# Splitting the next expert's weights in two steps in a routed mixture-of-experts stage

## The chip, the cores and the metric

The kernel runs on one core of a Trainium2 chip. The metric is the device time of one execution in microseconds (us); lower is better. The engines are PE (matrix products), DVE (vector), ACT (scalar), POOL (GpSimd) and SP, which here only issues DMAs.

## What is computed

Three parts follow one another: an mLSTM-like attention over 2 x 768 tokens, a dense mixture of four experts, and a routed mixture of eight experts. The change lies in the last one:

```python
def _moe2_ref(x, w_gate, w1, w2, capacity):
    N, D = x.shape                      # 1536, 320
    E = w_gate.shape[1]                 # 8
    logits = x @ w_gate
    expert_idx = np.argmax(logits, axis=1)
    ...                                 # gate_w: softmax probability of the chosen expert
    disp = np.zeros((E, capacity, D))   # capacity 384
    ...                                 # each token is copied to the next free row of its expert
    h = np.maximum(np.einsum('ecd,edf->ecf', disp, w1), 0.0)   # F = 1024
    y = np.einsum('ecf,efd->ecd', h, w2)
    ...                                 # out[i] = gate_w[i] * y[expert, row]
```

## The kernel before

**Precision by splitting.** Products run in a reduced format. Each operand is therefore held as a high part and a low part (value less high part), and three products are summed: high x high, low x high, high x low. The weights are split on the chip, each expert's while the expert before it is computed.

**Staging.** SP loads the weights of an expert in four pieces into `stage` (704 KB each, one buffer per piece), and a piece is loaded again as soon as POOL has counted it done on `w_ready`. Per piece p the split has these steps, in order of dependence:

- ACT, `w_to_hi`, two parts: the high part of w1 (L762, 128x768) and of w2 (L765, 128x640). Part number 2p is w1, 2p + 1 is w2.
- DVE, `w_tail`: the low part of a corner of w1, in place (L1151, 64x256), and with `w2_share` the low part of the first of the piece's two w2 tiles (L1155, 128x320). Both read `stage` and a high part, both in SBUF. It counts on `w_tail_done`.
- POOL, `w_to_lo`: waits for `w_tail_done`, then subtracts the rest of w1 (L897, 128x512) and, with `skip=1`, the other w2 tile (L905, 128x320), and counts on `w_ready`. PE waits for `w_ready` of piece p ahead of up tile 2p of the next expert.

**One routed expert.** Buffers alternate by parity (even, odd). PE makes 8 up tiles (f = 0 to 7, eight products each, L509 to L512), into three PSUM banks by turns: from f = 3 it waits until DVE has made h_lo of tile f - 3. ACT takes each tile as h_hi (L770), DVE as h_lo (L1186). At f = 3, 5 and 7 (`SLOT_STEPS`) PE also transposes a tile of the next expert's token rows (L638), which ACT (L833) and DVE (L1310) take over; after the last of them DVE waits for `out_sent` of the expert before and copies gates and token numbers (L1317, L1318). Then come the down products, 24 for each tile of 128 tokens, in the order of `TILE_ORDER` (2, 1, 0). DVE evicts each tile (L1332), POOL sends it with an indirect DMA (L1022). The three sends stand on POOL behind the four pieces of the next expert's weights. Tiles with no tokens are left out on PE, by a count in a register; DVE and POOL go through all three in every case, and PE signals the missing ones at once (a transpose, L678, stands in for one). With at most two tiles of tokens the up products are 256 columns wide, else 384.

In this run the experts, numbered here from 0, have 3, 1, 1, 1, 3, 3, 2 and 2 tiles. The routed stage's first up product starts at 468.66 us.

**The order of the work around the change** is written out by hand: each engine runs its own list, and a step stands where the code puts it. On DVE the steps of the weights stand after f = 1, 3, 5 and 7 (`W_STEPS`), on ACT one part after each f.

Of the kernel before, what the change touches and what calls it, by code (L numbers as in the profile page):

```python
# [41 lines left out]
def build_kernel(nc, gates, o_tok, q_t, qk_t, kv_tok, probs, w_moe1, w_moe2, w_gate, out, capacity):  # L42
# [8 lines left out]
    E1 = w_moe1.shape[0]  # L51
    E2 = w_moe2.shape[0]
    PIECES, STAGE = w_moe1.shape[1], w_moe1.shape[3]
# [5 lines left out]
    PF = F // PIECES  # L59
# [21 lines left out]

    SLOT_STEPS = (3, 5, 7)

    W_STEPS = (1, 3, 5, 7)

    SHIFTED, CHOSEN, SLOTS = 2, 5, 14
    LAST1 = BLOCKS1 - 1
# [14 lines left out]
    with ExitStack() as ctx:  # L102
# [126 lines left out]
        def xs_bank(e, par, n):  # L229


            if isinstance(e, int) and e == 0:
                return bank[7 - n]
            return bank[7 - (par + n) % 2]
# [473 lines left out]
        def _(act):  # L708
# [48 lines left out]
            def w_to_hi(x, w, p, part):  # L757


                if part == 0:  # L760
                    act.wait_ge(stage_in[p], 16 * x + 16)
                    act.activation(w1_hi[w][:, :, p * PF:(p + 1) * PF],  # L762
                                   stage[:, p, 0:KT * PF].rearrange("p (k f) -> p k f", k=KT), ACT.Copy).then_inc(w_hi_done, 1)
                else:
                    act.activation(w2_hi[w][:, p * PK:(p + 1) * PK, :],  # L765
                                   stage[:, p, KT * PF:STAGE].rearrange("p (k d) -> p k d", k=PK), ACT.Copy).then_inc(w_hi_done, 1)

            def hidden_hi(g, f):
                act.wait_ge(h_psum, 8 * g + (f + 1))
                act.activation(h_hi[:, f, :], ps_h[f % 3][:, 0:BLOCK], ACT.Relu).then_inc(h_hi_done, 1)  # L770
# [44 lines left out]
            e = E1 - 1  # L815
# [15 lines left out]
            def slots_to_hi(e, par, n):  # L831
                act.wait_ge(xs_psum, 3 * e + (n + 1))
                act.activation(xs_hi[par][:, :, n * P:(n + 1) * P], xs_bank(e, par, n)[:, 0:XD].rearrange("p (k t) -> p k t", k=KT),  # L833
                               ACT.Copy).then_inc(xs_hi_done, 1)

            def routed(e, par, last):
                for f in range(FT):
                    hidden_hi(e + G1, f)
                    if not last:
                        if f in SLOT_STEPS:  # L840
                            slots_to_hi(e + 1, 1 - par, SLOT_STEPS.index(f))
                        w_to_hi(e + (E1 + 1), 1 - par, f // 2, f % 2)

            for n in range(NT):
                slots_to_hi(0, 0, n)
            with act.Fori(0, E2 // 2 - 1) as i:
                routed(2 * i, 0, False)
                routed(2 * i + 1, 1, False)
            routed(E2 - 2, 0, False)
            routed(E2 - 1, 1, True)  # L850

# [185 lines left out]
        def _(dve):  # L1037
# [108 lines left out]
            def w_tail(x, w, p, cols, w2_share=False):  # L1146


                dve.wait_ge(w_hi_done, 8 * x + (2 * p + 1))
                hi = w1_hi[w][TAIL:P, 2, cols]  # L1150
                op = dve.tensor_tensor(hi, stage[TAIL:P, p, 2 * PF:3 * PF], hi.bitcast(F32), ALU.subtract)  # L1151
                if w2_share:
                    dve.wait_ge(w_hi_done, 8 * x + (2 * p + 2))
                    raw = stage[:, p, KT * PF:KT * PF + X]
                    op = dve.tensor_tensor(w2_lo[w][:, p * PK, :], raw, w2_hi[w][:, p * PK, :].bitcast(F32), ALU.subtract)  # L1155
                op.then_inc(w_tail_done, 1)
# [27 lines left out]
            def hidden_lo(g, f):  # L1184
                dve.wait_ge(h_hi_done, 8 * g + (f + 1))
                dve.scalar_tensor_tensor(h_lo[:, f, :], ps_h[f % 3][:, 0:BLOCK], 0.0, h_hi[:, f, :].bitcast(F32),  # L1186
                                         ALU.max, ALU.subtract).then_inc(h_done, 1)
# [86 lines left out]
            e = E1 - 1  # L1274
# [32 lines left out]
            def slots_to_lo(e, par, n):  # L1307
                cols = slice(n * P, (n + 1) * P)
                dve.wait_ge(xs_hi_done, 3 * e + (n + 1))
                dve.tensor_tensor(xs_lo[par][:, :, cols], xs_bank(e, par, n)[:, 0:XD].rearrange("p (k t) -> p k t", k=KT),  # L1310
                                  xs_hi[par][:, :, cols].bitcast(F32), ALU.subtract).then_inc(xs_done, 1)
                if n == NT - 1:
                    for k in range(NT):
                        dve.wait_ge(x_slot_in[par][k], 8 * e + (16 - 8 * par))

                    dve.wait_ge(out_sent[par], 24 * e - 24 * par)
                    dve.tensor_copy(gate_s[par][:], x_slot[par][:, :, GATE]).then_inc(meta_done, 1)  # L1317
                    dve.tensor_copy(token_s[par][:], x_slot[par][:, :, TOKEN]).then_inc(meta_done, 1)  # L1318

            def routed(e, par, last):  # L1320
                for f in range(FT):
                    hidden_lo(e + G1, f)
                    if not last:
                        if f in SLOT_STEPS:
                            slots_to_lo(e + 1, 1 - par, SLOT_STEPS.index(f))
                        if f in W_STEPS:
                            p = W_STEPS.index(f)
                            w_tail(e + (E1 + 1), 1 - par, p, slice(p * PF, (p + 1) * PF), w2_share=True)
                dve.wait_ge(meta_done, 2 * e + 2)
                for k, n in enumerate(TILE_ORDER):  # L1330
                    dve.wait_ge(y_psum, 3 * e + (3 * G1 + k + 1))
                    dve.tensor_scalar(y_out[par][:, n, :], ps_y[n][:, 0:X], gate_s[par][:, n:n + 1], None,  # L1332
                                      ALU.mult).then_inc(y_free, 1)

            for n in range(NT):
                slots_to_lo(0, 0, n)
            routed(0, 0, False)
            routed(1, 1, False)
            with dve.Fori(1, E2 // 2 - 1) as i:
                routed(2 * i, 0, False)  # L1340
                routed(2 * i + 1, 1, False)
# [59 lines left out]
```

## Time and profile before

| | us |
|---|---|
| median of 3 runs | 618.19 |
| the runs | 614.89, 619.23, 618.19 |
| the profiled execution, its own time | 620.88 |
| its span, first to last instruction | 619.1 |
| mean granted clock of PE over the span | 0.988 |

All rows below are from the profiled execution. The granted clock is 1.00 at 2.4 GHz and 0.50 at 1.2 GHz. A timeline row gives start, duration, engine, line of the code, operation, tile written <- tiles read, shapes, and in brackets the idle time before it and what ended it. PE rows overlap, since matrix products are pipelined; the distance between starts is what one costs.

### The profile page before, as it was taken

To read this page: it belongs to the slowest core of one execution; us is meant where nothing else is said; L and a number is where in the kernel's file an instruction comes from. 1 tells how busy PE (TensorE), PEld (TensorE's weight loads), DVE (VectorE), ACT (ScalarE), POOL (GpSimd) and SP (SyncE) were. 2 spreads that over 40 slices of the span, in tenths; PEclk is the share of its full clock that TensorE was granted. 3 is DMA by queue.
4 is the path that set the end of the run, shared out by engine and by line. 5 is a ranking of instruction groups with operands and counts; after the bars stand their busy time and mean duration, and the time that the engine had idled before them with its cause. 6 is when DMAs were issued, how large, how long until landed. Compare 5 with 4: busy or idle time off the path is not lost.

```text
span 619.1 us, 10721 instructions
## 1 busy us (share of the span) xinstructions
PE 585.3 (95%) x3847; PEld 571.0 (92%) x3847; DVE 284.9 (46%) x607; ACT 215.3 (35%) x468; POOL 212.6 (34%) x238
## 2 busy tenths in 40 slices
PE   0999999999999999999999999999988998899996
PEld 0877889999999999999999999999977998899996
DVE  7378876223322332332233232443434499855472
ACT  5344564213311321331132133131204286555341
POOL 9656539111101101110110121312331567764461
PEclk9999999999999999999999999999987999899999
DMA  6497634951011101101110110211123747764400
GB/s 193 112 231 180 164 146 138 365 213 47 0 47 48 47 0 47 47 1 47 47 47 0 48 47 1 86 42 45 60 70 107 237 156 238 246 220 143 158 16 18
DMA packets 25910, 63.50 MB, mean 103 GB/s; under 512 B 3310, under 2 KB 15543, under 8 KB 25876
## 3 DMA queue, kind: packets, MB, share of 16 engines
q1 hardware_dynamic: 23956, 58.98, 29.8%
q0 software_dynamic: 1920, 4.07, 1.8%
q8 instruction: 21, 0.34, 0.2%
q14 instruction: 13, 0.11, 0.1%
HBM read 52.16 MB, written 13.11 MB: 105 GB/s over the span
## 4 chain that ended last, share of the span: by engine, by line
PE 83%; POOL 4%; issue 3%; DVE 3%; ACT 3%; DMA 2%; SPq 1%; POOLq 0%; DVEq 0%; ACTq 0%
PE bank L509 27%; PE bank L524 9%; PE bank L525 9%; PE bank L526 9%; PE bank L512 5%; PE bank L511 4%; PE bank L667 3%; PE bank L666 3%; PE bank L665 3%; PE bank L447 2%; PE bank L475 2%; PE bank L579 1%; PE bank L568 1%; ACT h_hi L770 1%; POOL c_select L867 1%
## 5 line engine op out<-in xcount | busy, mean ns | idle before, releaser
L770 ACT ACTIVATE h_hi<-bank 128x384 fp32r<-128x384 f32 x192 | 94.7, 493 | 312.6 <-PE bank L512 311.9
L1186 DVE SCALAR_TENSOR_TENSOR h_lo<-bank,h_hi 128x384 fp32r<-128x384 f32 x192 | 105.7, 556 | 131.9 <-ACT h_hi L770 130.9
L897 POOL TENSOR_TENSOR w_lo_odd<-stage,w_hi_odd 128x512 fp32r<-128x512 f32 x24 | 31.4, 1307 | 149.0 <-DVE w_hi_odd L1151 119.6
L897 POOL TENSOR_TENSOR w_lo_even<-stage,w_hi_even 128x512 fp32r<-128x512 f32 x24 | 31.4, 1309 | 132.7 <-DVE w_hi_even L1151 119.6
L509 PE MATMUL bank<-xt_hi,w_hi_even 128*128 (+2 forms) x192 | 65.2, 340 | 3.4 <-DVE h_lo L1186 2.1
L509 PE MATMUL bank<-xt_hi,w_hi_odd 128*128 128x384 f32 (+2 forms) x192 | 63.6, 331 | 2.3 <-DVE h_lo L1186 2.3
L1195 DVE SCALAR_TENSOR_TENSOR acc<-bank,prob,acc 128x320 f32 (+1 forms) x36 | 19.8, 551 | 95.8 <-PE bank L526 92.9
L509 PE MATMUL bank<-xt_lo,w_hi_even 128*128 (+2 forms) x192 | 63.5, 331 | 0.0
L509 PE MATMUL bank<-xt_hi,w_lo_even 128*128 (+2 forms) x192 | 63.5, 331 | 0.0
L509 PE MATMUL bank<-xt_lo,w_hi_odd 128*128 128x384 f32 (+2 forms) x192 | 61.8, 322 | 0.0
L509 PE MATMUL bank<-xt_hi,w_lo_odd 128*128 128x384 f32 (+2 forms) x192 | 61.7, 322 | 0.0
L524 PE MATMUL bank<-w_hi_odd,h_hi 128*128 128x320 f32 x192 | 59.9, 312 | 0.0
L524 PE MATMUL bank<-w_hi_even,h_hi 128*128 128x320 f32 x192 | 59.4, 309 | 0.1
L525 PE MATMUL bank<-w_lo_odd,h_hi 128*128 128x320 f32 x192 | 59.3, 309 | 0.0
L526 PE MATMUL bank<-w_hi_even,h_lo 128*128 128x320 f32 x192 | 59.3, 309 | 0.0
L526 PE MATMUL bank<-w_hi_odd,h_lo 128*128 128x320 f32 x192 | 59.3, 309 | 0.0
L525 PE MATMUL bank<-w_lo_even,h_hi 128*128 128x320 f32 x192 | 59.3, 309 | 0.0
L509 PEld LDWEIGHTS bank<-xt_hi,w_hi_even 128*128 128x128 f32 x192 | 36.8, 192 | 4.4 <-DVE h_lo L1186 2.6
L509 PEld LDWEIGHTS bank<-xt_hi,w_hi_odd 128*128 128x128 f32 x192 | 36.1, 188 | 2.9 <-DVE h_lo L1186 2.8
L730 ACT ACTIVATE dmat<-bank,cols 128x128 f32<-128x128 f32 x96 | 27.4, 370 | 28.7 <-PE bank L434 26.1
L509 PEld LDWEIGHTS bank<-xt_lo,w_hi_even 128*128 128x128 f32 x192 | 36.9, 192 | 0.0
L509 PEld LDWEIGHTS bank<-xt_hi,w_lo_even 128*128 128x128 f32 x192 | 36.7, 191 | 0.0
(180 smaller groups left out, 1349.1 us busy)
## 6 DMA issues: line engine op xcount, KB each, us to landing
stage<-w_moe SPq DMA_DIRECT2D x48, 704.0 KB, 4.1
slot_rows<-empty_row SPq DMA_DIRECT2D x1, 4632.0 KB, 19.6
x_slot<-slot_rows SPq DMA_DIRECT2D x24, 193.0 KB, 4.4
qk_rows<-qk_t SPq DMA_DIRECT2D x12, 360.0 KB
kv<-kv_tok SPq DMA_DIRECT2D x12, 324.0 KB
q_diag<-q_t SPq DMA_DIRECT2D x36, 60.0 KB
sig<-o_tok SPq DMA_DIRECT2D x2, 960.0 KB, 6.2
out<-empty_row SPq DMA_DIRECT2D x2, 960.0 KB, 17.2
```

Source lines behind the costliest of these rows:

```text
L509: pe.matmul(dst, wk[w][:, k, cols], xk(k), start=(n == 0), stop=False)
L511: pe.matmul(dst, w1_hi[w][:, 2, cols], xh(2), start=False, stop=False)
L512: pe.matmul(dst, w1_hi[w][:, 2, cols], xl(2), start=False, stop=True).then_inc(h_psum, 1)
L524: pe.matmul(ps_y[n][:, 0:X], h_hi[:, f, rows], w2_hi[w][:, f, :], start=(f == 0), stop=False)
L525: pe.matmul(ps_y[n][:, 0:X], h_hi[:, f, rows], w2_lo[w][:, f, :], start=False, stop=False)
L526: mm = pe.matmul(ps_y[n][:, 0:X], h_lo[:, f, rows], w2_hi[w][:, f, :], start=False, stop=(f == FT - 1))
L665: pe.matmul(ps_y[n][:, 0:X], h_hi[:, f, rows], w2_hi[par][:, f, :], start=False, stop=False)
L730: op = act.activation(dmat[b][:, h, :], src[:, n * P:(n + 1) * P], ACT.Exp, bias=cols3[:, c, b * HEADS + h:b * HEADS + h + 1])
L770: act.activation(h_hi[:, f, :], ps_h[f % 3][:, 0:BLOCK], ACT.Relu).then_inc(h_hi_done, 1)
L897: return pool.tensor_tensor(w1_lo[w][:, :, cols], raw1[:, 0:2, :], w1_hi[w][:, 0:2, cols].bitcast(F32), ALU.subtract)
L1186: dve.scalar_tensor_tensor(h_lo[:, f, :], ps_h[f % 3][:, 0:BLOCK], 0.0, h_hi[:, f, :].bitcast(F32), ALU.max, ALU.subtract).then_inc(h_done, 1)
L1195: op = dve.scalar_tensor_tensor(acc[:, tile, 0:X], ps_y[n][:, 0:X], share, acc[:, tile, 0:X], ALU.mult, ALU.add)
```

## The change

The four steps of DVE and the eight parts of ACT for the next expert's weights are placed anew. During the up products ACT does parts 0, 1 and 2 (after f = 0, 2, 4) and DVE the step of piece 0 (after f = 4). ACT does parts 3 to 7 in a row after the last up tile. DVE does the steps of pieces 1, 2 and 3 between the output tiles, each ahead of its wait for a tile of down products. The lists of PE, POOL and SP stay as they are.

```diff
--- before.py
+++ after.py
@@ -81,7 +81,8 @@
 
     SLOT_STEPS = (3, 5, 7)
 
-    W_STEPS = (1, 3, 5, 7)
+    W_UP_ACT = {0: 0, 2: 1, 4: 2}
+    W_UP_DVE = 4
 
     SHIFTED, CHOSEN, SLOTS = 2, 5, 14
     LAST1 = BLOCKS1 - 1
@@ -839,7 +840,11 @@
                     if not last:
                         if f in SLOT_STEPS:
                             slots_to_hi(e + 1, 1 - par, SLOT_STEPS.index(f))
-                        w_to_hi(e + (E1 + 1), 1 - par, f // 2, f % 2)
+                        if f in W_UP_ACT:
+                            w_to_hi(e + (E1 + 1), 1 - par, W_UP_ACT[f] // 2, W_UP_ACT[f] % 2)
+                if not last:
+                    for part in range(len(W_UP_ACT), 2 * PIECES):
+                        w_to_hi(e + (E1 + 1), 1 - par, part // 2, part % 2)
 
             for n in range(NT):
                 slots_to_hi(0, 0, n)
@@ -1318,16 +1323,18 @@
                     dve.tensor_copy(token_s[par][:], x_slot[par][:, :, TOKEN]).then_inc(meta_done, 1)
 
             def routed(e, par, last):
+                def next_tail(p):
+                    if not last:
+                        w_tail(e + (E1 + 1), 1 - par, p, slice(p * PF, (p + 1) * PF), w2_share=True)
                 for f in range(FT):
                     hidden_lo(e + G1, f)
-                    if not last:
-                        if f in SLOT_STEPS:
-                            slots_to_lo(e + 1, 1 - par, SLOT_STEPS.index(f))
-                        if f in W_STEPS:
-                            p = W_STEPS.index(f)
-                            w_tail(e + (E1 + 1), 1 - par, p, slice(p * PF, (p + 1) * PF), w2_share=True)
+                    if f == W_UP_DVE:
+                        next_tail(0)
+                    if not last and f in SLOT_STEPS:
+                        slots_to_lo(e + 1, 1 - par, SLOT_STEPS.index(f))
                 dve.wait_ge(meta_done, 2 * e + 2)
                 for k, n in enumerate(TILE_ORDER):
+                    next_tail(k + 1)
                     dve.wait_ge(y_psum, 3 * e + (3 * G1 + k + 1))
                     dve.tensor_scalar(y_out[par][:, n, :], ps_y[n][:, 0:X], gate_s[par][:, n:n + 1], None,
                                       ALU.mult).then_inc(y_free, 1)
```

On DVE, expert 0, before: the four steps (L1151 and L1155) stand among the h_lo operations, and the three evictions follow in one row.

```order
L1186 SCALAR_TENSOR_TENSOR h_lo<-bank,h_hi 128x384 x2
L1151 TENSOR_TENSOR w_hi_odd<-stage,w_hi_odd 64x256
L1155 TENSOR_TENSOR w_lo_odd<-stage,w_hi_odd 128x320
...
L1186 SCALAR_TENSOR_TENSOR h_lo<-bank,h_hi 128x384 x2
L1310 TENSOR_TENSOR xt_lo<-bank,xt_hi 128x3x128
L1317 COPY gate_s<-x_slot 128x3
L1318 CAST token_s<-x_slot 128x3
L1151 TENSOR_TENSOR w_hi_odd<-stage,w_hi_odd 64x256
L1155 TENSOR_TENSOR w_lo_odd<-stage,w_hi_odd 128x320
L1332 TENSOR_SCALAR acc<-bank,gate_s 128x320 x3
L1186 SCALAR_TENSOR_TENSOR h_lo<-bank,h_hi 128x384 x2
```

The same place of DVE's list now (lines are shifted by five, L1332 is L1339):

```order
L1322 COPY gate_s<-x_slot 128x3
L1323 CAST token_s<-x_slot 128x3
L1156 TENSOR_TENSOR w_hi_odd<-stage,w_hi_odd 64x256
L1160 TENSOR_TENSOR w_lo_odd<-stage,w_hi_odd 128x320
L1339 TENSOR_SCALAR acc<-bank,gate_s 128x320
L1156 TENSOR_TENSOR w_hi_odd<-stage,w_hi_odd 64x256
L1160 TENSOR_TENSOR w_lo_odd<-stage,w_hi_odd 128x320
L1339 TENSOR_SCALAR acc<-bank,gate_s 128x320
L1156 TENSOR_TENSOR w_hi_odd<-stage,w_hi_odd 64x256
L1160 TENSOR_TENSOR w_lo_odd<-stage,w_hi_odd 128x320
L1339 TENSOR_SCALAR acc<-bank,gate_s 128x320
L1191 SCALAR_TENSOR_TENSOR h_lo<-bank,h_hi 128x384 x4
```

The place after the last up tile holds piece 1 now, where it held piece 3; pieces 2 and 3 stand between the evictions, all ahead of the next expert's first h_lo.

On ACT, the end of the up products of expert 0, before (`xt_hi` is here the buffer of the next expert's token rows):

```order
L762 ACTIVATE w_hi_odd<-stage 128x3x256
...
L770 ACTIVATE h_hi<-bank 128x384
...
L833 ACTIVATE xt_hi<-bank 128x3x128
L765 ACTIVATE w_hi_odd<-stage 128x640
...
L770 ACTIVATE h_hi<-bank 128x384
```

And now:

```order
L771 ACTIVATE h_hi<-bank 128x384
...
L834 ACTIVATE xt_hi<-bank 128x3x128
L766 ACTIVATE w_hi_odd<-stage 128x640
L763 ACTIVATE w_hi_odd<-stage 128x3x256
L766 ACTIVATE w_hi_odd<-stage 128x640
L763 ACTIVATE w_hi_odd<-stage 128x3x256
L766 ACTIVATE w_hi_odd<-stage 128x640
```

Where part 7 stood alone between two experts, parts 3 to 7 stand together.

## Rows read from the trace of the kernel before

**Rows 1.** The page, part 1: busy time of each engine.

```profile
PE 585.3 (95%) x3847; PEld 571.0 (92%) x3847; DVE 284.9 (46%) x607; ACT 215.3 (35%) x468; POOL 212.6 (34%) x238
```

**Rows 2.** Timeline of PE, expert 2. Columns: start us, us, engine, line, operation, what it writes and reads.

```profile
506.46 0.28 PE L509 MATMUL bank<-xt_hi,w_hi_even 128*128 128x256 f32 x1
...
509.35 0.49 PE L638 MATMUL bank<-ident,x_slot 128*128 128x128 f32 x3
...
509.59 0.36 PE L509 MATMUL bank<-xt_hi,w_hi_even 128*128 128x256 f32 x1
...
513.81 0.49 PE L638 MATMUL bank<-ident,x_slot 128*128 128x128 f32 x3
...
516.39 0.39 PE L509 MATMUL bank<-xt_hi,w_hi_even 128*128 128x256 f32 x1 [2.09 <-DVE h_lo L1186]
...
517.45 0.27 PE L678 MATMUL bank<-ident,h_hi 128*128 128x128 f32 x1
...
521.09 0.28 PE L509 MATMUL bank<-xt_hi,w_hi_odd 128*128 128x256 f32 x1
```

**Rows 3.** Timeline of DVE and POOL in the same expert.

```profile
507.38 1.46 DVE L1332 TENSOR_SCALAR acc<-bank,gate_s 128x320 f32<-128x320 f32 x3
...
512.89 2.98 DVE L1155 TENSOR_TENSOR w_lo_odd<-stage,w_hi_odd 128x320 fp32r<-128x320 f32 x1
...
515.79 1.01 DVE L1186 SCALAR_TENSOR_TENSOR h_lo<-bank,h_hi 128x384 fp32r<-128x384 f32 x2
...
512.42 0.98 POOL L1022 DMA_INDIRECT out<-acc,token_s  x1 [0.30 <-issue]
...
513.41 1.29 POOL L897 TENSOR_TENSOR w_lo_odd<-stage,w_hi_odd 128x512 fp32r<-128x512 f32 x1
...
514.67 0.85 POOL L905 TENSOR_TENSOR w_lo_odd<-stage,w_hi_odd 128x320 fp32r<-128x320 f32 x1
...
515.95 1.30 POOL L897 TENSOR_TENSOR w_lo_odd<-stage,w_hi_odd 128x512 fp32r<-128x512 f32 x1 [0.44 <-DVE w_lo_odd L1155]
```

**Rows 4.** Timeline of PE in expert 3; busy time, PEclk, DMA share and GB/s of its down products.

```profile
532.10 0.29 PE L678 MATMUL bank<-ident,h_hi 128*128 128x128 f32 x1
...
537.28 0.34 PE L509 MATMUL bank<-xt_hi,w_hi_even 128*128 128x384 f32 x1
...
532.10:537.20 5.10, 5.10 (x27) 5.10 (x26) 5.04 (x11) 1.50 (x3) 3.17 (x4) 0.67 0.77 266
```

**Rows 5.** Timeline of four engines at the end of expert 0's up products.

```profile
483.39 0.31 PE L657 MATMUL bank<-w_hi_even,h_hi 128*128 128x320 f32 x1
...
482.26 0.84 ACT L762 ACTIVATE w_hi_odd<-stage 128x768 fp32r<-128x768 f32 x1
...
484.35 0.74 ACT L765 ACTIVATE w_hi_odd<-stage 128x640 fp32r<-128x640 f32 x1
...
484.11 0.56 DVE L1186 SCALAR_TENSOR_TENSOR h_lo<-bank,h_hi 128x384 fp32r<-128x384 f32 x1 [0.66 <-ACT h_hi L770]
...
485.34 0.42 DVE L1151 TENSOR_TENSOR w_hi_odd<-stage,w_hi_odd 64x256 fp32r<-64x256 f32 x1
...
485.78 0.49 DVE L1155 TENSOR_TENSOR w_lo_odd<-stage,w_hi_odd 128x320 fp32r<-128x320 f32 x1
...
486.35 1.30 POOL L897 TENSOR_TENSOR w_lo_odd<-stage,w_hi_odd 128x512 fp32r<-128x512 f32 x1 [1.13 <-DVE w_lo_odd L1155]
...
487.61 0.89 POOL L905 TENSOR_TENSOR w_lo_odd<-stage,w_hi_odd 128x320 fp32r<-128x320 f32 x1
```

**Rows 6.** Timeline of PE in experts 1 and 4.

```profile
501.21 0.49 PE L638 MATMUL bank<-ident,x_slot 128*128 128x128 f32 x3
...
501.78 0.39 PE L509 MATMUL bank<-xt_hi,w_hi_odd 128*128 128x256 f32 x1
...
541.70 0.42 PE L509 MATMUL bank<-xt_hi,w_hi_even 128*128 128x384 f32 x1
```

**Rows 7.** Timeline of POOL, the last send.

```profile
614.90 0.97 POOL L1022 DMA_INDIRECT out<-acc,token_s  x1 [2.55 <-DVE acc L1332]
```


## Prediction

> **What bounds the kernel now.** I read the page first: PE is busy for 585.3 us [rows 1] of the 619.1 us span, DVE and POOL for less than half. So time is to be had only where PE stands still or runs slowly, and only in the routed stage, which the diff touches. The timeline of PE there is a chain without gaps, but for three kinds of places.
>
> First, expert 2, which has one tile of tokens. From its first up product at 506.46 to its first down product at 517.45 are 10.99 us, and in them lies one wait [rows 2]. The transposes of the slots start at 513.81 and PE goes on at 516.39, 2.58 us later; where nothing holds it, it goes on after 0.24 us (509.35 to 509.59). So 2.34 us are lost, put down to h_lo on DVE. The same gap stands in expert 3, the next of one tile, 2.52 us long.
>
> Why DVE is late is in its own timeline [rows 3]: a w_lo subtraction (L1155), 0.49 us elsewhere [rows 5], took 2.98 us from 512.89 to 515.87. POOL was at work without a break from 512.42 through its two subtractions of the same weights until 515.52, and DVE ended 0.35 us behind it. An operation of DVE whose inputs both lie in SBUF stands still until POOL is idle. Operations that read PSUM do not: the two h_lo from 515.79 took their usual 1.01 us beside POOL's row at 515.95.
>
> Second, after the gap of expert 3 the clock falls. Its down products take 5.18 us (532.10 to 537.28) at a mean granted clock of 0.67 [rows 4]; the same products of expert 2, 517.45 to 521.09, take 3.64 us. That is 1.5 us for one fall from 2.4 to 1.2 GHz. Of two gaps of the same kind, one was followed by a fall.
>
> Third, a wait of 0.57 less 0.24, 0.33 us, at the last slot transpose of expert 1 [rows 6], and one of 0.28 us like it in expert 6. In all the before loses 2.34 + 2.52 + 1.5 + 0.33 + 0.28 = 7.0 us to what the change touches.
>
> **What goes.** During the up products DVE now meets one weight step (after f = 4) instead of four, and ACT three parts instead of eight. The step at f = 3 that was held for 2.98 us is gone from there, and with it all 7.0 us, if nothing comes in its place. No work is added; instructions, bytes and DMAs are the same.
>
> **What comes.** Three weight steps of DVE now stand between the evictions of the expert, ahead of the next expert's first h_lo. I work out when that h_lo comes, in us after T, the start of the down products. The row pattern is the end of expert 0 [rows 5], with T = 483.39. There h_lo 7 starts at +0.72, the weight step at +1.95 (L1151) and +2.39 (L1155), which ends at +2.88; POOL follows at +2.96 and ends at 487.61 + 0.89, +5.11. In the changed kernel piece 1 stands in this place and keeps these times. Then:
>
> Eviction 1 starts when L1155 frees DVE, about +2.80, and takes 0.46 of DVE's time (1.46 us for three with the tail of the last) [rows 3]. In an expert of one tile its wait is met at once, since PE's stand-in transpose signals it.
>
> Step 2 is reached at +3.26. POOL has been on piece 1 since +2.96 and ends at +5.11. By the rows of 512.89 DVE is held until then: L1151 ends about +5.41, L1155 +5.92. POOL takes piece 2 from +6.00 to +8.15.
>
> Eviction 2, then step 3 at +6.30: held until +8.15, done at +8.96. Eviction 3 starts at +8.88, and h_lo 0 of the next expert at +9.34. PE resumes 0.60 us after such an h_lo starts (515.79 to 516.39): +9.94. POOL ends piece 3 at +11.19.
>
> PE wants this h_lo for its fourth up tile, since three banks rotate. With one tile of down products (3.64) and three up tiles with the transposes (506.46 to 509.59, 3.13) that is +6.77. So PE waits 9.94 - 6.77 = 3.17 us, at f = 3 and no more at f = 7. In expert 2: 3.17 for 2.34, +0.83. In expert 3: 3.17 for 2.52, +0.65. Expert 4 has three tiles and slower up tiles, 4.42 us to its fourth (537.28 to 541.70) [rows 4, 6], but follows an expert of one tile: it wants h_lo at 3.64 + 4.42 = 8.06 and gets it at 9.94, a new gap of 1.88 us.
>
> The other borders are covered. After an expert of three tiles PE has 10.5 us of down products, and the chain of 9 us fits in. After two tiles (expert 6) the next fourth tile is wanted near +10, where I find 9.94; that cover is thin. Expert 1 and 6 gain their 0.33 and 0.28.
>
> Clock: two gaps longer than the one of 2.5 us behind which it fell. I take one fall in each, two instead of one, +1.5; the third gap of 1.88 us is shorter than the 2.34 behind which it did not fall.
>
> Sum: 0.83 + 0.65 + 1.88 - 0.33 - 0.28 + 1.5 = +4.25 us. The profiled execution took 620.88 us, 2.7 over the median of 618.19; by it the changed kernel is at 625.1, and set on the median at 622.4.
>
> **ACT and the queues.** ACT's five late parts follow its last hidden and slot work, from +0.96 [rows 5]. With 0.84 for a w1 and 0.74 for a w2 part, the last ends by +0.96 + 3 x 0.74 + 2 x 0.84 = +4.86. Step 2 has its parts by +3.3 and step 3 by +4.9, both while DVE is held anyway, and the next expert asks ACT only after +4.9. They cost nothing here; if DVE were not held, step 3 would wait for them until +4.4 or so. On POOL three sends are queued behind piece 3: from about +11.3, 12.6 and 13.9, with piece 0 of the next weights behind them. The wait for out_sent at f = 7 then gets close. The last send of all started 614.90 [rows 7] and the span ended 4.2 us later, so a send is done by +18.1 at the latest; DVE asks at the next T (+3.64 + 8.65 + 3.17 = +15.46) plus 1.7, +17.1. Between nothing and 1.0 us may come of this per expert of one tile; I take nothing, since a fall of the clock pushes T back by 1.5. SP's load of a stage piece waits for POOL, and piece 0 comes late by some tenths for ACT's first part, at a time when DVE is the later one.
>
> **A rule beside the rows.** The rows show DVE held across the border between two subtractions of POOL (514.67). The Trainium skill, SBUF — State Buffer, section "SBUF: two separate sides", says that GpSimd and a DVE operation with two SBUF inputs share a port pair under an exclusive lock, held for the whole instruction of whoever starts first. The trace agrees that the loser stands still. Held for one instruction only, DVE would come in after the first subtraction, which is the next rival.
>
> **Rival 1, hand-over.** DVE gets in when POOL ends its first subtraction (+4.22). Step 2 ends at +5.03, POOL's second half runs to +5.92, step 3 ends at +6.73, h_lo 0 starts at +7.11, PE resumes at +7.71. Then expert 2 waits 0.94 us (-1.40), expert 3 as much (-1.58), expert 4 not at all, experts 1 and 6 give 0.61 and no clock falls (-1.5): -5.1, 613.1 us. Against it: twice (experts 2 and 3) DVE did not get in at such a border. With no hold at all, the full 7.0 us come back: 611.2. Against that stand all long rows of L1155 and L1151.
>
> **Rival 2, slower: the clock falls behind every gap.** Its place is expert 4, where a gap of 1.88 us is new, and its price one more fall, +1.5. It decides if PE's idle time there is enough for the gate, as 2.5 us were once and 2.3 once were not. And if the median run before had no fall, which the 614.89 us of one run makes possible, all three count: 618.19 + 2.75 + 3 x 1.5 = 625.4.
>
> **Rival 3, nothing moves.** Holds only change places, the gaps stay near 2.4 us, as where POOL's work starts later than I think: 618.
>
> **How the numbers follow.** The forecast has 0.56, rival 2 0.20, hand-over 0.14, no hold 0.04, nothing moves 0.06. Likeliest: 622.4. The range reaches from the hand-over (613) to a little above rival 2 (626.5), for the 1 us of out_sent; what is left out below is no hold and part of the hand-over's scatter. About 1% is what a measurement of this kernel tells from no change, 612.0 to 624.4. Faster by over 1%: no hold and half of the hand-over, less a rest, 0.11. Slower: most of rival 2 and the upper part of the forecast, 0.27. Within: 0.62.
>
> **What the changed profile would show.** L1151 between the evictions of experts 1, 2 and 3 at about 2.2 us each; PE's wait for h_lo at the fourth up tile of experts 2, 3 and 4 (about 3.2, 3.2, 1.9 us less the transposes), none at the eighth; two stretches of half clock; POOL's sends at +11. The forecast is wrong if those L1151 last 1.3 us or less, if ACT comes later than +5, or if the clock stays up.

## The result, and the profile after

The changed kernel takes 621.86 us (median of 11 runs, 619.74 to 623.92), the kernel before beside it 618.40 (11 runs, 614.89 to 620.29). The ratio is 1.0063, with a 95% interval of 1.0041 to 1.0086: slower by 0.6%, some 3.5 to 3.9 us. The profiled execution took 621.65 us with a span of 619.9.

Part 1 of the page, which answers to [rows 1], tells little of it: PE is busy for 1.4 us more, DVE for 1.6, and the counts of instructions are the same.

```profile
PE 586.7 (95%) x3847; PEld 572.9 (92%) x3847; DVE 286.5 (46%) x607; ACT 217.9 (35%) x468; POOL 213.5 (34%) x238
```

The timeline of PE shows where it stands still, and answers to [rows 2, 4, 6]. T of expert 1, the start of its down products, is now 500.80.

```profile
500.80 0.27 PE L679 MATMUL bank<-ident,h_hi 128*128 128x128 f32 x1
...
507.30 0.49 PE L639 MATMUL bank<-ident,x_slot 128*128 128x128 f32 x3
510.08 0.58 PE L510 MATMUL bank<-xt_hi,w_hi_even 128*128 128x256 f32 x1 [2.29 <-DVE h_lo L1191]
...
523.53 0.49 PE L639 MATMUL bank<-ident,x_slot 128*128 128x128 f32 x3
526.40 0.38 PE L510 MATMUL bank<-xt_hi,w_hi_odd 128*128 128x256 f32 x1 [2.38 <-DVE h_lo L1191]
...
541.23 0.49 PE L639 MATMUL bank<-ident,x_slot 128*128 128x128 f32 x3
542.75 0.44 PE L510 MATMUL bank<-xt_hi,w_hi_even 128*128 128x384 f32 x1 [1.03 <-DVE h_lo L1191]
```

There are three gaps, each at the fourth up tile: 2.78, 2.87 and 1.52 us between transposes and product, less the usual 0.24, so 2.54, 2.63 and 1.28. None is left at the eighth tile, where [rows 2] had one of 2.34. Expert 1's up products take 8.50 us (before 8.89), expert 6's 8.61 (before 8.89).

DVE from expert 1 to 2, with the weight steps (L1156 and L1160, once L1151 and L1155) between the evictions (L1339); it answers to [rows 3, 5].

```profile
504.14 1.16 DVE L1156 TENSOR_TENSOR w_hi_even<-stage,w_hi_even 64x256 fp32r<-64x256 f32 x1
505.32 1.07 DVE L1160 TENSOR_TENSOR w_lo_even<-stage,w_hi_even 128x320 fp32r<-128x320 f32 x1
506.31 0.54 DVE L1339 TENSOR_SCALAR acc<-bank,gate_s 128x320 f32<-128x320 f32 x1
506.88 1.15 DVE L1156 TENSOR_TENSOR w_hi_even<-stage,w_hi_even 64x256 fp32r<-64x256 f32 x1
508.05 1.05 DVE L1160 TENSOR_TENSOR w_lo_even<-stage,w_hi_even 128x320 fp32r<-128x320 f32 x1
...
509.49 1.47 DVE L1191 SCALAR_TENSOR_TENSOR h_lo<-bank,h_hi 128x384 fp32r<-128x384 f32 x3
```

And POOL in the same stretch (L902 and L910 are its two subtractions, once L897 and L905).

```profile
503.73 1.30 POOL L902 TENSOR_TENSOR w_lo_even<-stage,w_hi_even 128x512 fp32r<-128x512 f32 x1 [1.94 <-DVE w_lo_even L1160]
504.98 1.06 POOL L910 TENSOR_TENSOR w_lo_even<-stage,w_hi_even 128x320 fp32r<-128x320 f32 x1
506.47 1.28 POOL L902 TENSOR_TENSOR w_lo_even<-stage,w_hi_even 128x512 fp32r<-128x512 f32 x1 [0.43 <-DVE w_lo_even L1160]
507.71 1.05 POOL L910 TENSOR_TENSOR w_lo_even<-stage,w_hi_even 128x320 fp32r<-128x320 f32 x1
...
514.01 0.98 POOL L1027 DMA_INDIRECT out<-acc,token_s  x1 [0.30 <-issue]
```

Read the two together. DVE asks for L1156 at 504.14, while L902 runs; L902 ends at 505.03 and L1156 at 505.30. POOL's L910, 0.88 elsewhere, takes 1.06: it stood while L1156 ran. DVE's L1160 asks at 505.32, stands until L910 ends at 506.04, and ends at 506.39. Here the engines take turns, one instruction each, so DVE is held twice in a step, each time for the rest of one instruction of POOL. The pattern repeats at 506.88.

The windows of two stretches of PE: busy time by engine, then the mean granted clock, DMA share and GB/s.

```profile
510.10:513.50 3.40, 3.40 (x16) 3.40 (x16) 1.64 (x4) 0.87 (x2) 2.95 (x4) 0.50 0.85 263
...
527.20:530.60 3.40, 3.40 (x18) 3.40 (x17) 1.55 (x4) 1.85 (x4) 2.65 (x4) 0.51 0.88 323
```

Right behind the first two gaps the clock is at 1.2 instead of 2.4 GHz for 3.4 us. The kernel before had one such stretch in these experts [rows 4]. The other up products of expert 2 go at full clock, and all of them, without the gap, take 12.66 - 2.54 = 10.12 us against 8.50 in expert 1: 1.6 us for this fall.

From the start of expert 1's up products to the start of expert 7's down products are 112.26 us before (493.95 to 606.21) and 114.68 after (492.30 to 606.98), +2.42. The spans of the two executions differ by 0.8 only, because PE reached expert 1 1.65 us later in the one before.

### The profile page after: what moved, and what is told of

It is laid out like the page before. It is cut to its first block, busy times and chain, and to the rows that moved or that the text cites. A ratio compares the mean times of both kernels' runs of the same rounds, so it can differ in the third digit from the quotient of the medians.

```text
span 619.9 us, 10721 instructions
## 1 busy us (share of the span) xinstructions
PE 586.7 (95%) x3847; PEld 572.9 (92%) x3847; DVE 286.5 (46%) x607; ACT 217.9 (35%) x468; POOL 213.5 (34%) x238
## 4 chain that ended last, share of the span: by engine, by line
PE 82%; POOL 4%; DVE 3%; issue 3%; SPq 3%; DMA 3%; ACT 1%; POOLq 0%; DVEq 0%
PE bank L510 28%; PE bank L525 9%; PE bank L526 9%; PE bank L527 9%; PE bank L513 5%; PE bank L512 5%; PE bank L668 2%; PE bank L667 2%; PE bank L666 2%; PE bank L448 2%; PE bank L476 2%; SPq L318 2%; PE bank L580 1%; PE bank L639 1%; DMA g_rows<-g_saved_rows 1%
## 5 line engine op out<-in xcount | busy, mean ns | idle before, releaser
L902 POOL TENSOR_TENSOR w_lo_odd<-stage,w_hi_odd 128x512 fp32r<-128x512 f32 x24 | 31.3, 1303 | 158.8 <-DVE w_hi_odd L1156 119.6
L902 POOL TENSOR_TENSOR w_lo_even<-stage,w_hi_even 128x512 fp32r<-128x512 f32 x24 | 31.3, 1304 | 139.6 <-DVE w_hi_even L1156 119.6
```

The costliest lines, as they stand in the source:

```text
L902: return pool.tensor_tensor(w1_lo[w][:, :, cols], raw1[:, 0:2, :], w1_hi[w][:, 0:2, cols].bitcast(F32), ALU.subtract)
```

## The experiments

Medians and ratios are against the kernel before on the same chip (617.45 us over 23 runs for the first group of experiments, 617.58 over 25 for the second, 616.90 over 29 for the third). The diffs are against the changed kernel where nothing else is said.

### Is it POOL's subtractions that hold DVE?

**pool_short** gives POOL 16 columns instead of 512 and 320, so it leaves out most of the low parts that POOL makes.

```diff
+                if short:
+                    few = slice(p * PF, p * PF + 8)
+                    return pool.tensor_tensor(w1_lo[w][:, :, few], raw1[:, 0:2, 0:8],
+                                              w1_hi[w][:, 0:2, few].bitcast(F32), ALU.subtract)
...
+                d = slice(0, 16 if skip else X)
+                pool.tensor_tensor(w2_lo[w][:, tiles, d], raw2[:, :, d], w2_hi[w][:, tiles, d].bitcast(F32),
```

> The changed kernel, but POOL's two subtractions of each piece in the routed stage take 8 and 16 columns only, so the low parts of most weights stay old: this leaves out part of the computation. DVE, ACT, DMAs and all waits are the same. Hold theory: L1156 between the evictions takes 0.42 us, h_lo 0 starts near +6 us after the start of the down products, all three gaps at the fourth up tile go, no fall of the clock behind them: 7 us less than the changed kernel, ratio 0.992 to 0.997. If the place and number of DVE's steps make it late without POOL (rival), the gaps stay over 2 us.

612.16 us (6 runs), 0.9910 (0.9887 to 0.9933): a little more than expected. DVE's steps between the evictions:

```profile
504.48 0.42 DVE L1161 TENSOR_TENSOR w_hi_even<-stage,w_hi_even 64x256 fp32r<-64x256 f32 x1
504.92 0.49 DVE L1165 TENSOR_TENSOR w_lo_even<-stage,w_hi_even 128x320 fp32r<-128x320 f32 x1
...
507.21 1.01 DVE L1196 SCALAR_TENSOR_TENSOR h_lo<-bank,h_hi 128x384 fp32r<-128x384 f32 x2
```

Both are at the durations that nothing holds, the next expert's first h_lo comes 4.4 us behind the copies of expert 1's end (502.80) where the changed kernel has 7.0 (502.46 to 509.49), expert 2's up products take 8.59 us, and between 500 and 600 us no clock falls. The steps' new place costs nothing by itself; POOL's work beside them does. One wait is left that isn't theirs: at the end of expert 2 the copies wait 0.74 us for a send, and expert 3's up products take 9.32 us.

**pool_after_steps** lets POOL's pieces 1 to 3 wait for all four steps of DVE.

```diff
-                pool.wait_ge(w_tail_done, 4 * x + (p + 1))
+                pool.wait_ge(w_tail_done, 4 * x + max(p + 1, steps))
...
+                w1_to_lo(x, w, p, PIECES if skip and p else 0)
```

> The changed kernel, but POOL starts pieces 1 to 3 only when all four steps of DVE are done, so that POOL is idle while DVE works between the evictions. Hold theory: L1156 between the evictions takes 0.42 us again, not 1.16, h_lo 0 of the next expert starts near +6 us after the start of the down products, and the wait for h_lo ahead of the fourth up tile is gone; in its place PE waits for POOL's piece 1 ahead of the third up tile, about 2.3 us in experts 2 and 3 and 1.4 in expert 4, so the time stays within 0.3% of the changed kernel. If the number of steps alone made DVE late (rival), the wait for h_lo stays at 2 us or more.

632.36 us (5 runs), 1.0235 (1.0211 to 1.0260). The holds went as expected; the time did not. DVE, with the wait ahead of its copies in brackets:

```profile
504.80 0.17 DVE L1322 COPY gate_s<-x_slot 128x3 f32<-128x3 f32 x1 [3.97 <-DMA out<-acc,token_s]
...
505.07 0.42 DVE L1156 TENSOR_TENSOR w_hi_even<-stage,w_hi_even 64x256 fp32r<-64x256 f32 x1
```

PE in experts 2 and 3:

```profile
511.06 0.58 PE L510 MATMUL bank<-xt_hi,w_hi_even 128*128 128x256 f32 x1 [6.26 <-POOL w_lo_even L910]
...
528.62 0.38 PE L510 MATMUL bank<-xt_hi,w_hi_odd 128*128 128x256 f32 x1 [2.53 <-POOL w_lo_odd L910]
```

No step is held any more and the gap at the fourth up tile is gone; instead PE waits at the third for the weights that POOL now makes later. The 2.53 us of expert 3 are that alone. The 6.26 of expert 2 hold a second thing: the copies waited for a send that POOL had issued at 497.94 and that was done at 504.80, 6.9 us later. Expert 4 has the same again (PE waits 5.71 us, the copies 4.28 for the send of 535.49), and there and in expert 2 its up products are 6.2 and 5.0 us longer than in the changed kernel, with the clock at half behind both waits.

**steps_first** puts the three steps in a row ahead of the first eviction.

```diff
+                for p in range(1, PIECES):
+                    next_tail(p)
                 for k, n in enumerate(TILE_ORDER):
-                    next_tail(k + 1)
```

> The changed kernel, with DVE's steps of pieces 1, 2 and 3 in a row ahead of the first eviction instead of one ahead of each. DVE then asks for step 2 at about +2.85, before POOL starts piece 1 at +2.93. If the port goes to whoever asks first, for one instruction at a time, DVE loses at most one hold of 1.3 us and h_lo 0 starts at +6.5 to +7.5: gaps of 0.3 to 1.3 us in experts 2 and 3, none in expert 4, ratio 0.995 to 1.001. If only the total of work counts, the same gaps of 2.5, 2.4 and 1.3 us stay, ratio 1.006.

620.05 us (12 runs), 1.0036 (1.0014 to 1.0059); the gain that I expected did not come, though the ratio is a little under the 1.006 of the rival. DVE:

```profile
504.15 1.50 DVE L1160 TENSOR_TENSOR w_lo_even<-stage,w_hi_even 128x320 fp32r<-128x320 f32 x1
505.68 0.99 DVE L1156 TENSOR_TENSOR w_hi_even<-stage,w_hi_even 64x256 fp32r<-64x256 f32 x1
506.68 1.49 DVE L1160 TENSOR_TENSOR w_lo_even<-stage,w_hi_even 128x320 fp32r<-128x320 f32 x1
...
509.48 1.47 DVE L1191 SCALAR_TENSOR_TENSOR h_lo<-bank,h_hi 128x384 fp32r<-128x384 f32 x3
```

POOL:

```profile
503.76 1.54 POOL L902 TENSOR_TENSOR w_lo_even<-stage,w_hi_even 128x512 fp32r<-128x512 f32 x1 [1.94 <-DVE w_lo_even L1160]
505.26 1.12 POOL L910 TENSOR_TENSOR w_lo_even<-stage,w_hi_even 128x320 fp32r<-128x320 f32 x1
506.35 1.47 POOL L902 TENSOR_TENSOR w_lo_even<-stage,w_hi_even 128x512 fp32r<-128x512 f32 x1
507.78 1.11 POOL L910 TENSOR_TENSOR w_lo_even<-stage,w_hi_even 128x320 fp32r<-128x320 f32 x1
```

Turns again, in another order: L902 (1.54), L1160, L910 (1.12), L1156, L902 (1.47), L1160. h_lo 0 comes at 509.48 where the changed kernel has 509.49, and the gaps from transposes to product are 2.58, 2.59 and 1.42 us, where the changed kernel has 2.78, 2.87 and 1.52. What counts is how much subtraction of both engines lies ahead of h_lo, and hardly its order.

### Does ACT's new place matter?

**act_as_before** returns ACT's eight parts to the up tiles and leaves DVE as changed.

```diff
-                        if f in W_UP_ACT:
-                            w_to_hi(e + (E1 + 1), 1 - par, W_UP_ACT[f] // 2, W_UP_ACT[f] % 2)
-                if not last:
-                    for part in range(len(W_UP_ACT), 2 * PIECES):
-                        w_to_hi(e + (E1 + 1), 1 - par, part // 2, part % 2)
+                        w_to_hi(e + (E1 + 1), 1 - par, f // 2, f % 2)
```

> The changed kernel with ACT's eight parts put back as they were, one after each f; DVE keeps the new order. If DVE's weight steps between the evictions are late because POOL holds them (my theory), ACT's place does not matter: gaps ahead of the fourth up tile of experts 2, 3 and 4 of about 2.6, 2.5 and 1.4 us, and at most 0.3 us more at the last slot transposes; ratio to before 1.004 to 1.010. If the steps are late because ACT's five late parts come in a row (rival), these gaps shrink by over 1 us each and the time falls to that of before or under.

620.29 us (12 runs), 1.0034 (1.0015 to 1.0052): just below the range of the theory. PE:

```profile
514.29 0.39 PE L510 MATMUL bank<-xt_hi,w_hi_even 128*128 128x256 f32 x1 [2.44 <-DVE h_lo L1187]
...
529.74 0.39 PE L510 MATMUL bank<-xt_hi,w_hi_odd 128*128 128x256 f32 x1 [2.48 <-DVE h_lo L1187]
```

The gaps are there undiminished, so they are not ACT's. This trace has one fall of the clock in experts 2 and 3, not two. The two ratios' intervals overlap (1.0041 to 1.0086 for the whole change); whether ACT's move adds a tenth or two of a per cent is not settled.

### Do the sends matter?

In experts 1 to 3 two of POOL's three sends carry an empty tile. Two kernels leave these six out, one from before and one from the changed kernel; both have DVE's loop over the experts written out, so that its waits can be counted.

```diff
                 for k, n in enumerate(TILE_ORDER):
+                    if e in (1, 2, 3) and n:
+                        continue
...
-                    dve.wait_ge(out_sent[par], 24 * e - 24 * par)
+                    dve.wait_ge(out_sent[par], sends_ahead(e))
...
-            with dve.Fori(1, E2 // 2 - 1) as i:
+            for i in range(1, E2 // 2 - 1):
```

**before_fewer_sends**

> The kernel before, without the sends of the empty tiles of experts 1, 2 and 3 (six of 24 indirect DMAs; DVE's loop is written out for it). If the hold of 2.98 us came from POOL's unbroken run of sends and weight work (my theory), it shrinks to 1.4 us or less, both gaps ahead of the eighth up tile go (2.3 and 2.5 us) and no fall of the clock follows: about 6 us less, ratio 0.988 to 0.993. If the order on DVE alone makes them, the time stays, ratio 1.00.

613.96 us (6 runs), 0.9938 (0.9915 to 0.9962), just short of the size expected. In its trace expert 1, 2 and 3's up products take 8.88, 8.91 and 8.92 us: no gap, no fall. The longest step has an L1156 of 1.07 us, and no L1160 of 3 us is left.

**after_fewer_sends**

> The changed kernel, without the same six sends. In the changed kernel the sends stand behind piece 3, after the gap is made: the gaps ahead of the fourth up tile stay at 2.5, 2.4 and 1.3 us, the clock falls twice, ratio to before 1.004 to 1.009, 1.5% slower than the kernel before without these sends. If POOL's whole load made the gaps (rival), they go here too and the ratio is under 0.995.

617.72 us (12 runs), 1.0011 (0.9992 to 1.0030), less than expected. PE in expert 2:

```profile
506.43 0.49 PE L642 MATMUL bank<-ident,x_slot 128*128 128x128 f32 x3
509.22 0.39 PE L513 MATMUL bank<-xt_hi,w_hi_even 128*128 128x256 f32 x1 [2.30 <-DVE h_lo L1196]
```

The gap is as long as with all sends, as are the other two (2.87 and 1.52 us): in the changed kernel the sends make no gap. But in this profile the clock does not fall behind any of the three, and the mean clock of its 12 runs has a median of 0.990 for the changed kernel's 0.983. So with all the gaps of the changed kernel, but with the clock mostly up, this kernel is as fast as the kernel before; why the clock stays up without the six sends is not shown. Against before_fewer_sends it is 1.0061 (617.72 / 613.96), where 1.5% was expected.

**before_unrolled** writes the loop out in the kernel before and changes nothing else.

> The kernel before with DVE's loop over the experts written out, and nothing else: what the two kernels without the sends of empty tiles share beside their leaving out of sends. Theory (the sends, not the loop, gave before_fewer_sends its time): 0.998 to 1.002, with the gaps of experts 2 and 3 in place. Rival (the written-out loop gave part of it): 0.997 or below.

617.77 us (12 runs), 1.0015 (0.9997 to 1.0033). The loop gave nothing; the 0.6% of before_fewer_sends is the sends'. Expert 2 has its gap; that of expert 3 is half as long (PE waits 1.19 us for h_lo, 2.26 in the kernel before). The profile also shows the long hold again. DVE in experts 2 and 3:

```profile
508.28 0.42 DVE L1151 TENSOR_TENSOR w_hi_odd<-stage,w_hi_odd 64x256 fp32r<-64x256 f32 x1
508.72 2.98 DVE L1155 TENSOR_TENSOR w_lo_odd<-stage,w_hi_odd 128x320 fp32r<-128x320 f32 x1
...
524.68 1.59 DVE L1151 TENSOR_TENSOR w_hi_even<-stage,w_hi_even 64x256 fp32r<-64x256 f32 x1
```

POOL:

```profile
508.25 0.97 POOL L1022 DMA_INDIRECT out<-acc,token_s  x1 [0.30 <-issue]
509.23 1.29 POOL L897 TENSOR_TENSOR w_lo_odd<-stage,w_hi_odd 128x512 fp32r<-128x512 f32 x1
510.47 0.86 POOL L905 TENSOR_TENSOR w_lo_odd<-stage,w_hi_odd 128x320 fp32r<-128x320 f32 x1
...
523.84 1.32 POOL L897 TENSOR_TENSOR w_lo_even<-stage,w_hi_even 128x512 fp32r<-128x512 f32 x1
525.09 0.89 POOL L905 TENSOR_TENSOR w_lo_even<-stage,w_hi_even 128x320 fp32r<-128x320 f32 x1
```

In expert 2 it is the same picture as in [rows 3], to 0.01 us: L1155 starts 0.51 us ahead of L897, during the last send, and isn't let in between L897 and L905. In expert 3 L1151 asks at 524.68, when L897 has been running for 0.84 us, and it too gets in only behind L905, at 526.27; an L1151 of 1.95 us at 539.65 does the same. With the two of 2.98 us in the kernel before (512.89 and 527.54) these are five holds over both subtractions, and in all five L897 starts directly behind a send. In the changed kernel, where L902 starts after a wait for DVE, DVE is let in behind L902 each time. That is what the rows have in common; why it is so the runs don't show.

### What do the falls of the clock cost?

**gap_filled** gives PE sixteen products without use ahead of its wait at the fourth up tile of experts 2 and 3. PE's loop over the experts is written out for it; that alone was not run.

```diff
+                    def fill():
+                        for _ in range(16):
+                            pe.matmul(bank[7 - par][:, 0:X], w1_hi[par][:, 0, 0:P], w1_hi[par][:, 0, 0:X], start=True, stop=True)
```

> The changed kernel, with 16 products that nobody reads on PE ahead of its wait for h_lo at the fourth up tile of experts 2 and 3 (PE's loop is written out for it). They take 16 x 0.147 = 2.35 us, as long as PE stood idle there (2.29 and 2.38 us). If the falls of the clock at 510 and 527 us come from these gaps (my theory), they go and 2 x 1.5 us with them: ratio 1.000 to 1.003, no half clock between 500 and 540 us. If they fall by themselves (rival), the ratio stays at 1.006.

621.22 us (8 runs), 1.0060 (1.0036 to 1.0083): as the changed kernel, though the clock did what was expected. Windows, columns as above:

```profile
510.00:513.50 3.50, 3.50 (x33) 3.50 (x32) 2.97 (x7) 3.32 (x7) 2.81 (x3) 1.00 0.89 301
...
541.40:544.80 3.40, 3.40 (x13) 3.40 (x12) 1.15 (x3) 0.87 (x2) 2.63 (x4) 0.50 0.86 300
```

Expert 2's up products take 11.17 us instead of 12.66. Expert 3's take 12.45 instead of 12.73, though the clock stays up there too: the copies ahead of it wait 1.24 us for a send (517.18), all that follows on DVE and POOL is late by that, and PE waits 0.95 us for POOL at the third up tile. Expert 4's take 16.02 instead of 13.40: its gap has grown, and behind it the clock falls. PE there:

```profile
540.65 0.44 PE L512 MATMUL bank<-xt_hi,w_hi_even 128*128 128x384 f32 x1 [2.02 <-DVE h_lo L1196]
```

DVE and POOL, some us earlier:

```profile
533.01 0.17 DVE L1327 COPY gate_s<-x_slot 128x3 f32<-128x3 f32 x1 [0.99 <-DMA out<-acc,token_s]
...
528.82 1.11 POOL L1032 DMA_INDIRECT out<-acc,token_s  x1 [0.30 <-issue]
```

The copies wait 0.99 us for the send issued at 528.82, and every step and h_lo behind them comes later by that. Without the wait they would have come at 532.02, 3.2 us behind that send. In the changed kernel, which lost 1.6 us or more to the fall, they come 4.75 us behind it (535.10 for 530.35), and don't wait.

### Versions between the two

**two_and_two** has two steps of DVE during the up products, two ahead of the evictions, and ACT as before.

```diff
-                    if f == W_UP_DVE:
-                        next_tail(0)
+                    if f in (2, 6):
+                        next_tail((2, 6).index(f))
...
+                for p in (2, 3):
+                    next_tail(p)
```

> Meant to beat both: DVE's steps of pieces 0 and 1 after f = 2 and f = 6, of pieces 2 and 3 in a row ahead of the first eviction; ACT as in the kernel before. The step that was held for 2.98 us then stands behind every h_lo that PE waits for during the up products, and only two steps stand ahead of the next expert's first h_lo, which I expect at +6.4 to +7.5. Hold theory: gaps of up to 1.3 us in experts 2 and 3 in all, ratio 0.990 to 0.997. If POOL's load sets the pace of the experts of one tile wherever the steps stand (rival), gaps of 2 us or more stay, ratio 1.00.

616.40 us (12 runs), 0.9982 (0.9964 to 0.9999): faster than the changed kernel, and than the kernel before by little more than the interval. The gaps from transposes to product at the fourth up tile are 2.16 and 2.62 us long, which is the rival's sign, for the last step is held as before; expert 4's is gone (12.37 us for 13.40):

```profile
505.77 0.42 DVE L1152 TENSOR_TENSOR w_hi_even<-stage,w_hi_even 64x256 fp32r<-64x256 f32 x1
506.21 1.49 DVE L1156 TENSOR_TENSOR w_lo_even<-stage,w_hi_even 128x320 fp32r<-128x320 f32 x1
```

**before_w2_dve** is the kernel before with POOL's share of w2_lo on DVE.

```diff
-                    op = dve.tensor_tensor(w2_lo[w][:, p * PK, :], raw, w2_hi[w][:, p * PK, :].bitcast(F32), ALU.subtract)
+                    both = slice(p * PK, (p + 1) * PK)
+                    op = dve.tensor_tensor(w2_lo[w][:, both, :], raw, w2_hi[w][:, both, :].bitcast(F32), ALU.subtract)
...
-                        w_to_lo(e + (E1 + 1), 1 - par, p, skip=1)
+                        w1_to_lo(e + (E1 + 1), 1 - par, p).then_inc(w_ready, 1)
```

> The kernel before, but DVE takes POOL's share of w2_lo too (one instruction of 128x640 in place of 128x320), and POOL is left with w1_lo alone. Theory (the hold comes from the time that POOL and DVE together spend on subtractions with two inputs in SBUF): four steps of an expert took 4 x (0.42 + 0.49) on DVE and 4 x (1.27 + 0.88) on POOL, 12.2 us of the 12.3 that PE needs for an expert of one tile; now some 4 x (0.42 + 0.82) and 4 x 1.27, 10.0 us. The long hold of some 3 us at the fourth up tile can't come about, since no two subtractions stand in a row on POOL: longest L1156 or L1151 1.7 us, PE gaps in experts 2 and 3 under 1 us, ratio 0.990 to 0.996. Rival (DVE becomes the bound: with 4 x 0.33 us more it is busy for about 12.1 us of the 12.3, holds not counted): gaps of 1 us or more at both borders of every expert of one tile, ratio 1.000 or above.

614.58 us (12 runs), 0.9967 (0.9946 to 0.9988): faster, just outside the expected range. DVE in expert 2:

```profile
510.22 0.80 DVE L1151 TENSOR_TENSOR w_hi_odd<-stage,w_hi_odd 64x256 fp32r<-64x256 f32 x1
511.02 0.83 DVE L1156 TENSOR_TENSOR w_lo_odd<-stage,w_hi_odd 128x640 fp32r<-128x640 f32 x1
```

PE:

```profile
512.37 0.39 PE L509 MATMUL bank<-xt_hi,w_hi_even 128*128 128x256 f32 x1 [0.63 <-DVE h_lo L1187]
```

128x640 takes DVE 0.83 us where 128x320 took 0.49, so 0.34 us of DVE replace 0.88 of POOL. The hold of 2.98 is gone, the longest is some 0.4 (0.80 against 0.42), and experts 2 and 3 take 9.53 and 9.52 us. Of the gaps 0.9 us each are left; DVE has then been at work without a break since 507.29, with 0.4 us of it the hold of L1151, so the rest is DVE's own load.

**two_w2_dve** joins the last two.

> Two steps of DVE during the up products and two ahead of the evictions, as in two_and_two, and DVE takes POOL's share of w2_lo as in before_w2_dve. Theory (port time): the last two steps take about 4.0 us in all instead of 4.5, h_lo 0 of the next expert comes some 0.5 to 1.0 us earlier than in two_and_two (there +5.6 us after the first weight step at 503.5), PE gaps 1.2 to 1.7 us instead of 2.16 and 2.62, ratio 0.990 to 0.996. Rival (DVE is the bound): gaps as in two_and_two or longer, ratio 0.998 or above.

618.35 us (12 runs), 1.0032 (1.0005 to 1.0060): the rival. DVE's last step ahead of the evictions:

```profile
506.72 1.84 DVE L1157 TENSOR_TENSOR w_lo_even<-stage,w_hi_even 128x640 fp32r<-128x640 f32 x1
508.48 1.46 DVE L1337 TENSOR_SCALAR acc<-bank,gate_s 128x320 f32<-128x320 f32 x3
```

The last two steps took 3.38 us in two_and_two (504.24 to 507.62) and take 3.49 here (504.99 to 508.48). The shorter holds are eaten up by DVE's 0.34 us more in each, and by one more in each step ahead of them. The gaps from transposes to product are 2.44, 2.27 and 0.90 us (two_and_two 2.16, 2.62 and none), and this trace has two falls of the clock behind them, that of two_and_two one.

## Why the prediction was right, and where its terms were not

**The forecast.** 622.4 was forecast and 621.86 measured, slower by 0.6% with ratio and sign as worked out. The mechanism stands in its outline: holds moved from the eighth up tile to between the evictions, gaps at the fourth up tile of experts 2, 3 and 4, none at the eighth, none in experts 5 to 7, where more tiles of down products cover the chain. pool_short takes the holds away and with them all of the loss and more. That the number came within 0.5 us is partly luck: the sum was +4.25 us where the two traces differ by 2.42 in these experts, and the medians differ by 1.0 to 1.5 us more than the traces do, for a reason that is not found.

**The holds were sized too long.** This is the step "held until then", that is until POOL has done both its subtractions. DVE asked at T + 3.34 (forecast 3.26), but L1156 was through at +4.50 and L1160 at +5.59, where I had +5.41 and +5.92; the second step was through at +8.30 for +8.96. h_lo 0 came at +8.69 for +9.34, and PE resumed at +9.28 for +9.94. The gaps are 2.54, 2.63 and 1.28 us for 3.17, 3.17 and 1.88. The prediction named a sign for this, an L1151 between the evictions of 1.3 us or less (it is L1156 now), and with 1.16 us it is met: as to how long POOL holds DVE, the forecast was wrong by its own measure. I had made a rule ("stands still until POOL is idle") of the two holds of 2.98 us; the rows of L1151 between 0.85 and 1.08 us in the kernel before fit either rule, since DVE asks there when POOL is at its second subtraction. Rival 1 had the border right and what follows wrong: it let DVE's whole step in at one border (+7.71), where DVE gets one instruction. The truth lies between, nearer to the forecast. L1156 ends 0.27 us behind L902, and L1160 0.35 behind L910. The Trainium skill, SBUF — State Buffer, section "SBUF: two separate sides", has the lock held for one instruction. By these rows the trace agrees; by the five holds over both subtractions, in the kernel before and in before_unrolled, it doesn't.

**The sum by its terms.** On the two profiles: expert 2's gap +0.20 (forecast +0.83), expert 3's +0.11 (+0.65), expert 4's +1.28 (+1.88), expert 1 -0.39 (-0.33), expert 6 -0.28 (-0.28). The terms without the clock give +0.9 us where I had +2.75. The rest of the +2.42 between the two traces, 1.5 us, is one fall more, for which I had 1.5.

**The falls.** Two falls in experts 2 and 3 for one before, none behind the third gap: as forecast. The price was right too: behind the same gaps experts 2 and 3 take 12.66 and 12.73 us with a fall each, and 11.15 and 11.09 in after_fewer_sends without, so 1.5 and 1.6 us. What the traces don't settle is the median. The mean clock of a run has a median of 0.983 in the 11 runs of the changed kernel, and of 0.988 in the 23 runs of the kernel before beside the first group of experiments. A fall of 3.4 us at half clock lowers a mean over 620 us by 0.0027, so the median run has nearly two falls more, not one. But a mean doesn't say where they are. The two profiled executions have just these means, and in them one of the two lies in expert 2 or 3; the other lies between 27 and 33 us (mean clock 0.72 there, in the kernel before 1.00), long before the first changed instruction. The traces also scatter by more than the clock: before_unrolled, the kernel before but for a loop, takes 111.12 us from expert 1's up products to expert 7's down products, with one fall as well, where the profile of the kernel before took 112.26. So the changed kernel's 114.68 are +3.56 or +2.42, by which of the two they are set against. Rival 2's median run before without a fall is shown by neither of these two traces, and the fall that it has in expert 4 came in gap_filled and pool_after_steps alone, behind longer waits.

**No cost of ACT.** Forecast nothing, with the last part at +4.86; it ended at +4.41 (505.21), and act_as_before kept all the gaps. Right, to the 0.2% left open above.

**The wait for out_sent.** I gave it 0 to 1.0 us and took nothing, since a fall pushes T back. In the changed kernel it is nothing; in gap_filled, where the fall is gone, it is 0.99 at the end of expert 3 and 1.24 at the end of expert 2, where pool_short has 0.74. So where no fall pushes T back it is there, as worked out, but its bound was not right: I had a send done within 4.2 us, and in pool_after_steps one took 6.9.

**The thin cover** of expert 7 behind the two tiles of expert 6 held: its up products take 7.54 us, before 7.55.

**What stays open**: why DVE isn't let in between L897 and L905 in five cases; why the clock fell behind a gap in one kernel and not behind an equal one in another (2.30 us in after_fewer_sends, 2.29 in the changed kernel); and where the medians lose the 1.0 to 1.5 us that the two traces don't show.

## What to carry over

Count the time of all operations that need the shared access to SBUF, on both engines together, against the stage in which they lie: here four steps took 4 x (0.42 + 0.49 + 1.27 + 0.88) = 12.2 us, where PE needs 8.50 + 3.62 = 12.1 us for an expert of one tile, and with all sends none of the orders tried hid it. The sum is a warning, not a bound: before_fewer_sends has the same 12.2 us and no gap, with 2 x (0.98 + 0.30) = 2.6 us less of sends on POOL. So what else the slower engine has to do counts with it. Moving such work to another place moves the wait; taking it off the slower engine (before_w2_dve, 0.34 us for 0.88) or taking away what crowds it there (before_fewer_sends) gave time back. And when a wait of PE goes or comes, look at what the clock does behind it: here one fall more was 1.5 of the 2.4 us between the two traces. The mean clock of a run also counts falls that have nothing to do with the change, so look where they lie.

## What the runs showed of the hardware

- DVE and POOL, both with subtractions whose inputs lie in SBUF, take turns one instruction each in the changed kernel: L1156 1.16 us for 0.42, L1160 1.07 for 0.49, L910 1.06 for 0.88. The traced duration of an instruction holds the time for which it is held.
- Five holds in two kernels break this: where POOL's first subtraction came directly behind a send, DVE stood until the second was done too (three times 2.98 us, once 1.95, once 1.59).
- An indirect send of 128 rows was done 4.2 us after its issue in one case and 6.9 us in another, both in the routed stage.
- An indirect send of an empty tile costs POOL what a full one does: 0.98 us, and 0.30 to the next.
- Sixteen products without use kept the clock at 1.00 where it otherwise fell to 0.50, and the time was lost to the next waits in line.
- Equal gaps of PE (waits of 2.29 and 2.30 us) were followed by 3.4 us at half clock in one kernel and by none in another; such a fall cost 1.5 to 1.6 us.
